# Expert rounds of a routed feed-forward kernel: counts, digits, turns and two vector operations at other places

## The chip, the cores and the metric

The kernel runs on one core of one Trainium2 chip. The metric is the device time of one execution in microseconds (us); lower is better. TensorE (PE) multiplies matrices, VectorE (DVE) and ScalarE (ACT) work elementwise, GpSimd (POOL) also issues the indirect transfers, and SyncE (SP) issues plain transfers. Every engine runs its own instructions in the order in which they are written; between engines only semaphores order the work.

## The reference

```python
def reference(**kwargs):
    attn_out = _attn_ref(**attn_kwargs)              # linear attention, 4 x 8 heads x 768 tokens x 48
    x = attn_out ... reshape(3072, 384)
    x = _moe_ref(x=x, **moe_kwargs)                  # x @ w_in, leaky relu with slope alpha, @ w_out
    return _moe2_ref(x=x, **moe2_kwargs)

def _moe2_ref(x, w_gate, w1, w2):                    # N 3072, D 384, E 8 experts, F 1024
    cap = N // E                                     # 384 tokens for each expert
    order = np.argsort(-(x @ w_gate).flatten())
    for idx in order:                                # greedy: best (token, expert) pair first
        tok, e = (int(idx) // E, int(idx) % E)
        if assigned[tok] >= 0 or counts[e] >= cap:
            continue
        assigned[tok] = e
        counts[e] += 1
    for e in range(E):
        mask = assigned == e
        out[mask] = np.maximum(x[mask] @ w1[e], 0.0) @ w2[e]
```

The first two parts (attention and the first feed-forward layer) are not touched. This case is about the last part: 3072 tokens are handed out to 8 experts of 384 tokens each, and each expert is a feed-forward layer 384 -> 1024 -> 384.

## The kernel before

**Eight experts, one search ahead.** The greedy loop is replaced by eight searches. Search p finds which expert fills up next and at what threshold; its 384 tokens are then known, and are expert p of the stream. TensorE works on expert p while search p + 1 runs in the gaps. One such stretch is called a round: `body(new)` on TensorE, with `new` from 0 to 7. Round `new` carries search q = new + 1; search 7 (in round 6) is short, since only one expert is left.

**The stream.** A round has 48 places (`at` = 0 to 47). At each place TensorE issues one step of the stream, three matmuls with a moving size of 384 (L1312, L1313, L1314: each product is made of a high and a low float part). Groups of three places alternate between a hidden piece (`expert_hidden(p, f)`, x times w1, `xeh`/`xel` in the rows) and a back piece (`expert_back(p, f)`, hidden times w2, `gh`/`gl` in the rows), with f from 0 to 7. The stream lags by 15 places, so places 0 to 14 still belong to the expert before: place 0 starts the back piece of f = 4, place 3 the hidden piece of f = 6, place 6 the back piece of f = 5, and so on; place 15 starts the new expert's first hidden piece. After a hidden piece ACT makes the high part with a relu (`relu_hi`, L737), then VectorE the low part (`relu_lo`, L1113); the back piece of that f waits for it (`g2l_ready`).

**The search.** A search has six steps m = 1 to 6. In each VectorE compares all keys with 40 thresholds (the `grid`, L1203 or L1205), TensorE counts with 12 small matmuls (`count`, L1505), VectorE turns the counts into hits (`rest` L1210, `hits` L1211), TensorE makes one matmul of them (`digit`, L1552), and VectorE reads the threshold found (L1214). Only then can the next grid be made. After step 6 VectorE closes the search (`close`, with `running` L1223), TensorE makes `offsets` (L1556), VectorE the slots and the one-hot tiles `is_b` (L1147), TensorE `inverse` in two halves (L1564), VectorE the indices (`indices`, L1154). GpSimd then gathers the rows `xg` of the new expert with three indirect transfers (L589), and TensorE turns them (`turn_rows(new, a)`, a = 0 to 2, L1574) in the next round; ACT copies a turned piece to its high part (`rows_hi`, L743) and VectorE makes the low part `xel` (`rows_lo`, L1120). All three turned pieces of a round share one PSUM bank, so turn a waits for `rows_lo` of a - 1.

**What sets the order.** On TensorE, tables of places in `body`: `counts_at` and `digits_at` (one place for each of six steps), `offsets_at`, `inverses_at`, `turns_at`. At one place the order is count, digit, offsets, inverse, turn, and then the stream's step. On VectorE the order is written out in `route(p)`, and the low parts are fitted in by `while_counting(p, m)` (between a step's grid and its wait for the count) and `while_placing(p, m)` (between its hits and its wait for the digit):

```python
                    while_counting(p, level * V3 + n + 1)
                    dve.wait_ge(counts_done, m)
                    ...                              # rest, hits
                    while_placing(p, level * V3 + n + 1)
                    dve.wait_ge(digit_ready, m)
```

For p of 3 and more, `rows_lo(p - 1, 0)` stands in `while_counting` of step 2, `rows_lo(p - 1, 1)` in `while_placing` of step 2, and `rows_lo(p - 1, 2)` in `while_counting` of step 3. In these names the first number of a turned piece or a low part counts experts, and a search p works beside expert p - 1.

Of the kernel before, what the change touches and what calls it, by code (L numbers as in the profile page):

```python
# [32 lines left out]
def build(nc, rT, kT, rN, kN, v, wT, uR, w_in, w_out, alpha, w_gate, w1, w2, out):  # L33
# [3 lines left out]
    E, _, F2 = w1.shape  # L37
    KD = DM // P
    NF, NF2 = F // P, F2 // P
    NT = NCH * B  # L40
# [9 lines left out]
    with ExitStack() as ctx:  # L50
# [3 lines left out]
        def sem(name):  # L54
            return ctx.enter_context(nc.semaphore(name))
# [139 lines left out]
        onehot_ready, grid_ready, counts_done = sem("onehot_ready"), sem("grid_ready"), sem("counts_done")  # L195
# [84 lines left out]
        def hidden_h(p, f):  # L280

            return last_gh[:] if (p, f) == (E - 1, NF2 - 1) else gh[:, f % 2, 0:CAP]

        def hidden_l(p, f):

            return last_gl[:] if (p, f) == (E - 1, NF2 - 1) else gl[:, f % 2, 0:CAP]
# [511 lines left out]
        def _(dve):  # L798
# [137 lines left out]
            def over_experts(a):  # L936
                return a.unsqueeze(2).to_broadcast([P, a.shape[1], E])

            def over_tokens(a, n, m=NT):
                return a.unsqueeze(1).to_broadcast([P, m, n])  # L940
# [3 lines left out]
            def step(ins):  # L944

                ins.then_inc(route_step, 1)
                route_steps[0] += 1

            def hold(ins):

                step(ins)
                dve.wait_ge(route_step, route_steps[0])

            def front_best(js):

                hold(V.tensor_reduce(best[:, js], logits[:, js], AX_X, ALU.max))
                hold(V.tensor_tensor(onehot0[:, js], logits[:, js], over_experts(best[:, js]), ALU.is_equal))

            def front_rank(js):

                hold(V.tensor_tensor(ranked[:, js], onehot0[:, js], over_tokens(rev_ps, E, js.stop - js.start), ALU.mult))
                hold(V.tensor_reduce(rankmax[:, js], ranked[:, js], AX_X, ALU.max))
# [5 lines left out]
            def front_keys(js, done):  # L968

                V.tensor_tensor(onehot[:, js], ranked[:, js], over_experts(rankmax[:, js]), ALU.is_equal).then_inc(done, 1)  # L970
                hold(V.tensor_scalar(bits_s[:, js], best[:, js].bitcast(I32), 31, SIGN, ALU.arith_shift_right, ALU.bitwise_or))
                hold(V.tensor_tensor(bits_u[:, js], bits_s[:, js], best[:, js].bitcast(I32), ALU.bitwise_xor))
                step(V.tensor_copy(key_low[:, js], bits_u[:, js].bitcast(U16).rearrange("p (j h) -> p h j", h=2)[:, 0]))
# [136 lines left out]
            def relu_lo(p, f):  # L1110

                dve.wait_ge(g2h_ready, NF2 * p + f + 1)
                V.scalar_tensor_tensor(out=hidden_l(p, f), in0=banks[3 + f % 2][:, 0:CAP], scalar=0.0, in1=hidden_h(p, f).bitcast(F32),  # L1113
                                       op0=ALU.max, op1=ALU.subtract).then_inc(g2l_ready, 1)

            def rows_lo(p, a):

                dve.wait_ge(xgh_ready, NA * p + a + 1)
                rows = slice(a * P, (a + 1) * P)
                V.tensor_tensor(xel[:, p % 2, :, rows], turned_rows(p, a), xeh[:, p % 2, :, rows].bitcast(F32), ALU.subtract).then_inc(xgl_ready, 1)  # L1120
# [35 lines left out]
            def while_counting(p, m):  # L1156

                if p == 1 and m == 2:
                    rows_lo(0, 0)
                    rows_lo(0, 1)  # L1160
                if p == 1 and m == 4:
                    relu_lo(0, 0)
                if p == 2 and m == 2:
                    relu_lo(0, 6)
                    rows_lo(1, 0)
                if p == 2 and m == 3:
                    rows_lo(1, 2)
                    relu_lo(0, 7)
                if p == 2 and m == 6:
                    relu_lo(1, 1)  # L1170
                if p >= 3 and m == 1:
                    relu_lo(p - 2, 5)
                if p >= 3 and m == 2:
                    rows_lo(p - 1, 0)
                if p >= 3 and m == 3:
                    relu_lo(p - 2, 6)
                    rows_lo(p - 1, 2)
                if p >= 3 and m == 4:
                    relu_lo(p - 2, 7)
                if p >= 3 and m >= 5:  # L1180
                    relu_lo(p - 1, m - 5)

            def while_placing(p, m):

                if p == 1 and m == 2:
                    rows_lo(0, 2)
                if p == 2 and m == 4:
                    relu_lo(1, 0)
                if p >= 2 and m == 2:
                    rows_lo(p - 1, 1)  # L1190
                if p == 1 and m >= 5:
                    relu_lo(0, m - 4)
# [37 lines left out]
            def slots(p):  # L1230

                dve.wait_ge(running_ready, p + 1)
                dve.wait_ge(offsets_done, p + 1)
                step(V.scalar_tensor_tensor(out=sure_slot[:], in0=running[:, 0:NT], scalar=banks[5][:, 0:1], in1=sure_tie[:, 0:NT], op0=ALU.add, op1=ALU.mult))
                hold(V.scalar_tensor_tensor(out=tie_slot, in0=running[:, NT:2 * NT], scalar=banks[5][:, 1:2], in1=sure_tie[:, NT:2 * NT], op0=ALU.add, op1=ALU.mult))
                hold(V.tensor_tensor(slot, sure_slot[:], tie_slot, ALU.add))
# [14 lines left out]
            def route(p):  # L1251

                search(p, 0, key[:])
                hold(V.scalar_tensor_tensor(out=key2[:], in0=key[:], scalar=found[0], in1=key_low, op0=ALU.subtract, op1=ALU.add))
                search(p, 1, key2[:])
                close(p)
                slots(p)
                inversion(p)
                if p in (1, 2):
                    relu_lo(p - 1, 3)  # L1260
                inversion_b(p)
                if p >= 3:
                    relu_lo(p - 1, 3)
                dve.wait_ge(inverse_ready, 3 * p + 2)
                front_best(slice(0, NT))
                indices(p)
                front_rank(slice(0, NT))
                if p >= 1:
                    relu_lo(p - 1, 4)
                if p + 2 < E:  # L1270
                    front_keys(slice(0, NT), onehot_ready)
                survivors()
                if p + 2 < E:
                    start_key(slice(0, NT))
                if p == 1:
                    relu_lo(0, 5)
# [30 lines left out]
        def _(pe):  # L1307
# [308 lines left out]
            def body(new):  # L1616

                q = new + 1
                counts_at = ((2, 5, 18, 23, 27, 31), (7, 11, 15, 19, 23, 27), (3, 7, 12, 17, 21, 25))[new] if new < 3 else (2, 7, 11, 16, 21, 25)
                digits_at = ((4, 6, 19, 24, 28, 32), (9, 13, 16, 20, 24, 28), (5, 10, 14, 18, 22, 26))[new] if new < 3 else (4, 9, 13, 17, 22, 26)  # L1620
                offsets_at = (36, 32)[new] if new < 2 else 30
                inverses_at = ((44, 45), (40, 41))[new] if new < 2 else (38, 39) if new < E - 2 else (25, 26)
                turns_at = ((4, 4, 5), (9, 11, 13), (7, 9, 11))[new] if new < 3 else (5, 7, 10)
                busy_at = {0: 9, 2: 2, 4: 4, 5: 2, 6: 1, 7: 1} if new == 0 else {}
                for at in range(6 * NF2):
                    if q < E - 1:
                        for m in range(2 * V3):
                            if at == counts_at[m]:
                                count(q, m + 1)
                            if at == digits_at[m]:  # L1630
                                digit(q, m + 1)
                        if at == offsets_at:
                            offsets(q)
                        if at in inverses_at:
                            inverse(q, inverses_at.index(at))
                    elif q == E - 1:
                        if at == 2:
                            offsets(q)
                        if at in inverses_at:
                            inverse(q, inverses_at.index(at))  # L1640
                    for a in range(NA):
                        if at == turns_at[a]:
                            turn_rows(new, a)
                    busy(busy_at.get(at, 0), banks[0])
                    while done[0] < 6 * NF2 * new + at + 1 - BEGINS:
                        stream(done[0])
                        done[0] += 1
# [52 lines left out]
```

## Time and profile before

| | us |
|---|---|
| median of 3 runs | 809.49 |
| lowest, highest run | 808.98, 809.88 |
| span of the profiled execution | 808.1 |
| TensorE matmul busy in it | 770.3 |
| VectorE busy | 500.5 |
| GpSimd busy | 474.9 |
| ScalarE busy | 220.1 |

The profiled execution has no device time of its own beside its span; the span is what its first and last instruction enclose, and it lies 1.39 us below the median of the three runs. The stretch of the change begins at about 575 us. Times of places in a round are given by the trace's clock; a start of one three-matmul step to the next takes about 0.52 us where nothing is waited for.

### The profile page before, as it was taken

To read this page: it belongs to the slowest core of one execution; us is meant where nothing else is said; L and a number is where in the kernel's file an instruction comes from. 1 tells how busy PE (TensorE), PEld (TensorE's weight loads), DVE (VectorE), ACT (ScalarE), POOL (GpSimd) and SP (SyncE) were. 2 spreads that over 40 slices of the span, in tenths; PEclk is the share of its full clock that TensorE was granted. 3 is DMA by queue.
4 is the path that set the end of the run, shared out by engine and by line. 5 is a ranking of instruction groups with operands and counts; after the bars stand their busy time and mean duration, and the time that the engine had idled before them with its cause. 6 is when DMAs were issued, how large, how long until landed. Compare 5 with 4: busy or idle time off the path is not lost.

```text
span 808.1 us, 15970 instructions
## 1 busy us (share of the span) xinstructions
PE 770.3 (95%) x6320; PEld 649.6 (80%) x6320; DVE 500.5 (62%) x1038; ACT 220.1 (27%) x452; POOL 474.9 (59%) x471
## 2 busy tenths in 40 slices
PE   6899999999999999999999999939999999999997
PEld 4578888888888888888888888726887988989996
DVE  8877766556655565556655334477787777776221
ACT  1233322111211121112111211204244344353451
POOL 6899985555555555555554333107477775775871
PEclk8999999999999999999999999958999999999999
DMA  7865522222221222222000000014523605517401
GB/s 213 228 197 155 150 70 70 69 69 70 67 67 63 66 67 63 64 64 67 11 11 11 11 11 10 14 54 168 186 74 144 215 20 198 171 45 272 159 11 49
DMA packets 46569, 75.17 MB, mean 93 GB/s; under 512 B 6256, under 2 KB 31856, under 8 KB 46496
## 3 DMA queue, kind: packets, MB, share of 16 engines
q1 hardware_dynamic: 37776, 56.07, 22.1%
q10 hardware_dynamic: 5584, 8.46, 3.7%
q0 software_dynamic: 3136, 9.64, 3.4%
q8 instruction: 50, 0.82, 0.5%
q14 instruction: 23, 0.19, 0.1%
HBM read 64.71 MB, written 9.44 MB: 92 GB/s over the span
## 4 chain that ended last, share of the span: by engine, by line
PE 81%; DVE 11%; POOL 2%; issue 2%; ACT 2%; DMA 1%; SPq 0%; POOLq 0%; DVEq 0%; ACTq 0%
PE bank L1312 23%; PE bank L1314 22%; PE bank L1313 21%; PE bank L1329 3%; PE bank L1363 3%; PE bank L1346 2%; DVE grid L1205 2%; PE bank L1422 2%; PE bank L1505 2%; DVE grid L1203 1%; POOL gl L493 1%; PE bank L1564 1%; DVE both L860 1%; PE bank L1382 1%; DVE xel L1120 1%
## 5 line engine op out<-in xcount | busy, mean ns | idle before, releaser
L493 POOL TENSOR_TENSOR gl<-g,gh 128x512 fp32r<-128x512 f32 x96 | 128.2, 1336 | 202.4 <-ACT gh L667 202.2
L1003 DVE TENSOR_SCALAR q<-bank,alpha_sb 128x512 f32<-128x512 f32 x96 | 71.9, 749 | 146.2 <-PE bank L1314 146.0
L667 ACT CAST gh<-g 128x512 fp32r<-128x512 f32 x96 | 59.6, 621 | 335.4 <-PE bank L1314 298.8
L1312 PE MATMUL bank<-gh,wout_h 128*128 128x512 f32 x288 | 118.7, 412 | 1.2 <-DVE vs L887 0.4
L1312 PE MATMUL bank<-xTh,win_h 128*128 128x512 f32 x288 | 113.1, 393 | 0.3 <-DVE xTl L896 0.3
L1314 PE MATMUL bank<-gh,wout_l 128*128 128x512 f32 x288 | 112.8, 392 | 0.0
L1313 PE MATMUL bank<-gl,wout_h 128*128 128x512 f32 x288 | 112.4, 390 | 0.0
L1314 PE MATMUL bank<-xTh,win_l 128*128 128x512 f32 x288 | 112.2, 389 | 0.0
L1313 PE MATMUL bank<-xTl,win_h 128*128 128x512 f32 x288 | 112.0, 389 | 0.0
L599 POOL TENSOR_TENSOR w1l<-raw,w1h 128x384 fp32r<-128x384 f32 x64 | 65.1, 1016 | 38.4 <-ACT w2h L731 37.9
L1312 PE MATMUL bank<-xeh,w1h 128*128 128x384 f32 x192 | 69.6, 362 | 0.0
L1006 DVE SCALAR_TENSOR_TENSOR g<-bank,q 128x512 f32<-128x512 f32 x96 | 66.4, 691 | 3.3
L1312 PE MATMUL bank<-w2h,gh 128*128 128x384 f32 x189 | 68.0, 360 | 0.1
L1312 PEld LDWEIGHTS bank<-gh,wout_h 128*128 128x128 f32 x288 | 54.1, 188 | 14.7 <-POOL gl L493 2.6
L600 POOL TENSOR_TENSOR w2l<-raw,w2h 128x384 fp32r<-128x384 f32 x64 | 64.9, 1015 | 0.0
L1314 PE MATMUL bank<-xeh,w1l 128*128 128x384 f32 x192 | 64.7, 337 | 0.0
L1313 PE MATMUL bank<-xel,w1h 128*128 128x384 f32 x192 | 64.4, 336 | 0.0
L1313 PE MATMUL bank<-w2l,gh 128*128 128x384 f32 x189 | 63.8, 338 | 0.0
L1314 PEld LDWEIGHTS bank<-gh,wout_l 128*128 128x128 f32 x288 | 54.0, 188 | 12.1
L1314 PE MATMUL bank<-w2h,gl 128*128 128x384 f32 x189 | 63.7, 337 | 0.0
L1312 PEld LDWEIGHTS bank<-xTh,win_h 128*128 128x128 f32 x288 | 54.1, 188 | 11.8 <-DVE xTl L896 0.8
L1314 PEld LDWEIGHTS bank<-xTh,win_l 128*128 128x128 f32 x288 | 54.1, 188 | 11.5
(203 smaller groups left out, 1453.6 us busy)
## 6 DMA issues: line engine op xcount, KB each, us to landing
raw<-w SPq DMA_DIRECT2D x32, 768.0 KB
rt<-rT SPq DMA_DIRECT2D x48, 96.0 KB, 2.9
vs<-v SPq DMA_DIRECT2D x48, 96.0 KB, 3.0
vn<-v SPq DMA_DIRECT2D x24, 192.0 KB, 2.9
x2rows<-x2n SPq DMA_DIRECT2D x23, 192.0 KB, 1.9
kt<-kT SPq DMA_DIRECT2D x44, 96.0 KB, 2.5
kn<-kN SPq DMA_DIRECT2D x20, 192.0 KB, 2.5
rn<-rN SPq DMA_DIRECT2D x20, 192.0 KB, 2.6
```

Source lines behind the costliest of these rows:

```text
L493: nc.gpsimd.tensor_tensor(gl[:, f % 2], g[:, f % 2], gh[:, f % 2].bitcast(F32), ALU.subtract).then_inc(gl_ready, 1)
L599: nc.gpsimd.tensor_tensor(w1l[:, f], raw1[:, p % 2, :, f * P:(f + 1) * P], w1h[:, f].bitcast(F32), ALU.subtract).then_inc(wlo1_ready, 1)
L600: nc.gpsimd.tensor_tensor(w2l[:, f], raw2[:, p % 2, f, :], w2h[:, f].bitcast(F32), ALU.subtract).then_inc(wlo_ready, 1)
L667: nc.scalar.copy(gh[:, f % 2], g[:, f % 2]).then_inc(gh_ready, 1)
L1003: nc.vector.tensor_scalar(q[:, f % 2], h, 0.0, alpha_sb[:, f:f + 1], ALU.min, ALU.mult).then_inc(q_ready, 1)
L1006: nc.vector.scalar_tensor_tensor(out=g[:, f % 2], in0=h, scalar=0.0, in1=q[:, f % 2], op0=ALU.max, op1=ALU.add).then_inc(g_ready, 1)
L1205: V.scalar_tensor_tensor(out=grid[:, js, 0:R], in0=wide, scalar=found[level], in1=row, op0=ALU.subtract, op1=ALU.is_ge).then_inc(grid_read ...
L1312: nc.tensor.matmul(o, a_h, b_h, start=first, stop=False)
L1313: nc.tensor.matmul(o, a_h, b_l, start=False, stop=False)
L1314: return nc.tensor.matmul(o, a_l, b_h, start=False, stop=last)
L1329: mm = nc.tensor.matmul(score_bank(c, b, j)[halves(j), h * HT:(h + 1) * HT], kt[heads_in(j), b % 2, h], weights(c, b)[heads_in(j), j, h], ...
L1363: return nc.tensor.matmul(y_bank(c, b)[halves(j), cols], weights(c, b)[:, j, h], vs[:, b, j, cols], start=(h == 0), stop=(h == H - 1), ski ...
```

## The change

Four edits, all in the expert rounds. (1) In `route(p)`, the next search's keys (`front_keys`, four VectorE operations, L970 to L973) stand ahead of the low part of the fifth hidden piece, `relu_lo(p - 1, 4)`. This holds for every p from 1 to 5. (2) For searches 3 to 6, `relu_lo(p - 2, 7)`, the low part of the expert's last hidden piece (called the seventh in the change's short title, f = 7 here), moves from the count of step 4 to between the hits and the digit of step 3. (3) In rounds 2 to 5, counts, digits, offsets and inverses stand up to two places later. (4) The turns of round 2 stand one place later, and the first turn of rounds 3 to 6 one place earlier.

```diff
@@ while_counting
                 if p >= 3 and m == 3:
                     relu_lo(p - 2, 6)
                     rows_lo(p - 1, 2)
-                if p >= 3 and m == 4:
-                    relu_lo(p - 2, 7)
                 if p >= 3 and m >= 5:
                     relu_lo(p - 1, m - 5)
@@ while_placing
                 if p == 2 and m == 4:
                     relu_lo(1, 0)
+                if p >= 3 and m == 3:
+                    relu_lo(p - 2, 7)
@@ route
                 front_rank(slice(0, NT))
+                if p + 2 < E:
+                    front_keys(slice(0, NT), onehot_ready)
                 if p >= 1:
                     relu_lo(p - 1, 4)
-                if p + 2 < E:
-                    front_keys(slice(0, NT), onehot_ready)
                 survivors()
@@ body
-                counts_at = ((2, 5, 18, 23, 27, 31), (7, 11, 15, 19, 23, 27), (3, 7, 12, 17, 21, 25))[new] if new < 3 else (2, 7, 11, 16, 21, 25)
-                digits_at = ((4, 6, 19, 24, 28, 32), (9, 13, 16, 20, 24, 28), (5, 10, 14, 18, 22, 26))[new] if new < 3 else (4, 9, 13, 17, 22, 26)
-                offsets_at = (36, 32)[new] if new < 2 else 30
-                inverses_at = ((44, 45), (40, 41))[new] if new < 2 else (38, 39) if new < E - 2 else (25, 26)
-                turns_at = ((4, 4, 5), (9, 11, 13), (7, 9, 11))[new] if new < 3 else (5, 7, 10)
+                counts_at = ((2, 5, 18, 23, 27, 31), (7, 11, 15, 19, 23, 27), (4, 8, 12, 17, 21, 26))[new] if new < 3 else (2, 7, 12, 17, 21, 26)
+                digits_at = ((4, 6, 19, 24, 28, 32), (9, 13, 16, 20, 24, 28), (6, 10, 14, 18, 23, 28))[new] if new < 3 else (4, 9, 14, 18, 23, 28)
+                offsets_at = (36, 32)[new] if new < 2 else 31
+                inverses_at = ((44, 45), (40, 41))[new] if new < 2 else (39, 40) if new < E - 2 else (25, 26)
+                turns_at = ((4, 4, 5), (9, 11, 13), (8, 10, 12))[new] if new < 3 else (4, 7, 10) if new < E - 1 else (5, 7, 10)
```

The number of instructions on every engine stays as it was. Three places show the new order.

VectorE at the end of a search (edit 1), as a piece of the difference; L961 and L962 rank the experts for the next search, L1113 is the low part, L970 to L973 are the keys, and L1240 begins `survivors`:

```order
 L961 TENSOR_TENSOR ranked<-onehot,bank 128x192
 L962 TENSOR_REDUCE bank<-ranked 128x24
-L1113 SCALAR_TENSOR_TENSOR gl<-bank,gh 128x384
 L970 TENSOR_TENSOR onehot<-ranked,bank 128x192
 L971 TENSOR_SCALAR bits_s<-bank 128x24
 L972 TENSOR_TENSOR bits_u<-bits_s,bank 128x24
 L973 CAST bank<-bits_u 128x24
+L1113 SCALAR_TENSOR_TENSOR gl<-bank,gh 128x384
 L1240 TENSOR_SCALAR middle<-bank 128x24
 L1241 SCALAR_TENSOR_TENSOR middle<-bank,middle 128x24
```

The low part moved behind the four operations of the keys.

VectorE around steps 3 and 4 of searches 3 to 6 (edit 2), again as a piece of the difference; the first L1210 and L1211 are `rest` and `hits` of step 3, L1214 reads the threshold after the digit, L1203 is the grid of step 4:

```order
 L1210 TENSOR_TENSOR rest<-cap_c,bank 40x8
 L1211 TENSOR_TENSOR hits<-bank,rest 40x8
+L1113 SCALAR_TENSOR_TENSOR gl<-bank,gh 128x384
 L1214 TENSOR_REDUCE bank<-bank 128x1
 L1254 SCALAR_TENSOR_TENSOR key<-key,bank 128x24
 L1203 TENSOR_TENSOR grid<-key,bank 128x24x40
 L1207 SCALAR_TENSOR_TENSOR rev<-bank,rev 128x8
-L1113 SCALAR_TENSOR_TENSOR gl<-bank,gh 128x384
 L1210 TENSOR_TENSOR rest<-cap_c,bank 40x8
 L1211 TENSOR_TENSOR hits<-bank,rest 40x8
```

The low part now stands between the hits and the read of the threshold of step 3.

TensorE in round 2, search 3. Before, from the second turn (L1574) to the digit of step 2 (L1552) and the third turn; the three-row groups between are steps of the stream, and the count of step 3 comes one stream step after the last row:

```order
L1574 MATMUL bank<-id_wg,xg 128x128 x3
L1312 MATMUL bank<-xeh,w1h 128x384
L1313 MATMUL bank<-xel,w1h 128x384
L1314 MATMUL bank<-xeh,w1l 128x384
L1552 MATMUL bank<-hits,sized 128x8
L1312 MATMUL bank<-xeh,w1h 128x384
L1313 MATMUL bank<-xel,w1h 128x384
L1314 MATMUL bank<-xeh,w1l 128x384
L1574 MATMUL bank<-id_wg,xg 128x128 x3
```

The same stretch of the changed kernel, from the digit of step 2 to the count of step 3 (L1505) and the third turn:

```order
L1552 MATMUL bank<-hits,sized 128x8
L1574 MATMUL bank<-id_wg,xg 128x128 x3
L1312 MATMUL bank<-xeh,w1h 128x384
L1313 MATMUL bank<-xel,w1h 128x384
L1314 MATMUL bank<-xeh,w1l 128x384
L1312 MATMUL bank<-xeh,w1h 128x384
L1313 MATMUL bank<-xel,w1h 128x384
L1314 MATMUL bank<-xeh,w1l 128x384
L1505 MATMUL bank<-onehot,grid 128x16 x12
L1574 MATMUL bank<-id_wg,xg 128x128 x3
```

The second turn went from one stream step ahead of the digit to right behind it, and the third turn from one stream step ahead of the count to right behind it.

## Rows read from the trace of the kernel before

**Rows 1.** The page: span, and busy time of TensorE.

```profile
span 808.1 us, 15970 instructions
PE 770.3 (95%) x6320; PEld 649.6 (80%) x6320; DVE 500.5 (62%) x1038; ACT 220.1 (27%) x452; POOL 474.9 (59%) x471
```

**Rows 2.** Waits from 555 to 808 us: total us, times, longest us.

```profile
PEld bank L1505 <- DVE grid L1205: 4.5, 16, 0.7
```

**Rows 3.** Timeline at the end of round 0: start us, us, engine, line, operation, idle before.

```profile
575.89 0.56 DVE L1113 SCALAR_TENSOR_TENSOR gl<-bank,gh 128x384 fp32r<-128x384 f32 x1
576.37 0.34 DVE L970 TENSOR_TENSOR onehot<-ranked,bank 128x192 bf16<-128x192 f32 x1
577.15 0.17 DVE L1240 TENSOR_SCALAR middle<-bank 128x24 f32<-128x24 f32 x1
576.50 0.44 PE L1312 MATMUL bank<-w2h,gh 128*128 128x384 f32 x1
```

**Rows 4.** Timeline at the end of round 1.

```profile
606.91 0.34 DVE L1154 TENSOR_SCALAR idx<-bank 64x3 int32<-64x3 f32 x2 [1.57 <-PE bank L1564]
608.07 0.56 DVE L1113 SCALAR_TENSOR_TENSOR gl<-bank,gh 128x384 fp32r<-128x384 f32 x1
609.21 0.34 PE L1312 MATMUL bank<-w2h,gh 128*128 128x384 f32 x1
611.49 0.45 PE L1505 MATMUL bank<-onehot,grid 128*128 128x16 bf16 x12 [0.52 <-DVE grid L1203]
```

**Rows 5.** Timeline of round 2, steps 2 to 4 of search 3.

```profile
614.63 0.46 PE L1505 MATMUL bank<-onehot,grid 128*128 128x16 bf16 x12 [0.35 <-DVE grid L1205]
616.81 0.16 DVE L1211 TENSOR_TENSOR hits<-bank,rest 40x8 bf16<-40x8 f32 x1
616.73 0.52 PE L1574 MATMUL bank<-id_wg,xg 128*128 128x128 f32 x3 [0.21 <-DVE xel L1120]
617.79 0.56 DVE L1120 TENSOR_TENSOR xel<-bank,xeh 128x384 fp32r<-128x384 f32 x1 [0.82 <-ACT xeh L743]
618.47 1.22 DVE L1205 SCALAR_TENSOR_TENSOR grid<-key,bank 128x960 bf16<-128x960 f32 x1
619.74 0.46 PE L1505 MATMUL bank<-onehot,grid 128*128 128x16 bf16 x12 [0.20 <-DVE grid L1205]
623.29 0.46 PE L1505 MATMUL bank<-onehot,grid 128*128 128x16 bf16 x12
```

**Rows 6.** TensorE timeline of round 3, search 4; the last row opens round 4.

```profile
644.04 0.46 PE L1505 MATMUL bank<-onehot,grid 128*128 128x16 bf16 x12
650.63 0.34 PE L1314 MATMUL bank<-xeh,w1l 128*128 128x384 f32 x1
651.01 0.46 PE L1505 MATMUL bank<-onehot,grid 128*128 128x16 bf16 x12
654.41 0.46 PE L1505 MATMUL bank<-onehot,grid 128*128 128x16 bf16 x12
661.03 0.34 PE L1314 MATMUL bank<-w2h,gl 128*128 128x384 f32 x1
661.48 0.18 PE L1552 MATMUL bank<-hits,sized 65*128 65x8 bf16 x1
663.69 0.18 PE L1556 MATMUL bank<-running,before_b 128*128 128x2 bf16 x1
675.65 0.46 PE L1505 MATMUL bank<-onehot,grid 128*128 128x16 bf16 x12
```

**Rows 7.** TensorE timeline of round 6, at its second turn.

```profile
741.77 0.34 PE L1314 MATMUL bank<-w2h,gl 128*128 128x384 f32 x1
742.38 0.52 PE L1574 MATMUL bank<-id_wg,xg 128*128 128x128 f32 x3 [0.27 <-DVE xel L1120]
```

**Rows 8.** Gathered rows: the first gather of expert 4, and landing times of those recorded.

```profile
670.56 0.98 POOL L589 DMA_INDIRECT xg<-x2rows,idx  x1 [3.56 <-DVE idx L1154]
DMA to landing us min/median/max: 3.8/5.5/6.1
```

## The prediction, made before the changed kernel ran

> **What bounds the kernel now.** I read the page first: TensorE's matmuls are busy for 770.3 of 808.1 us [rows 1], so a change in the rounds counts only by what TensorE waits. Next the list of waits from 555 us on. It shows only short ones, the largest group being counts that wait for a grid, 4.5 us in 16 waits [rows 2]. Then the timelines, where I looked at start-to-start distances on TensorE: three matmuls of a stream step start 0.17 to 0.18 us apart, so any larger distance is an inserted matmul or a wait. Rounds 3, 4 and 5 are copies of each other: from the first count at 644.04 to the next round's at 675.65 are 31.61 us [rows 6]. In them TensorE waits before the count of step 3 (0.38 us from the matmul at 650.63 to 651.01, against 0.17: 0.21), by the same reading 0.24 before the count of step 4 at 654.41, about 0.08 before its digit, and 0.28 before the last digit (661.03 to 661.48, 0.45 against 0.17) [rows 6]. That is 0.8 us a round, the most that edit 3 can win there. The count and everything behind it stand in one chain: grid, count, hits, digit, read, next grid. A table that puts them later wins where TensorE came too early, and costs nothing as long as the chain keeps its own pace.
>
> **Edit 1, rounds 0 and 1: keys first.** At the end of round 0, VectorE makes the low part at 575.89, it ends at 576.45, and TensorE's back piece starts at 576.50 [rows 3]: TensorE is waiting for just this operation. The four key operations take from 576.37 to 577.15, 0.78 us [rows 3]. Put ahead, they delay the low part and so TensorE by 0.78. What VectorE does for the first grid is as long as before, and nothing later in round 1 waits for a clock of its own (grids, hits and turns all follow TensorE's count), so I take the whole 0.78 as lasting. The bounds are 0, if a later wait took it up, and 0.78. **+0.78.**
>
> At the end of round 1 the low part starts at 608.07 and the back piece runs at 609.21 [rows 4]. With keys first, the low part starts at 608.85, ends at 609.41, and TensorE starts at 609.46, 0.25 late, and 0.1 more for the refill that a first matmul behind a stall shows (0.28 to the next instead of 0.18). The first count then stands one place later. Before it was held to 611.49 by its grid [rows 4]; now four stream steps from 609.46 (0.63 and three of 0.53, the last of them place 3) bring it to 611.67, when the grid is done. The count is 0.18 later, but with one stream step more behind it. The 1.57 us that VectorE waits ahead of 606.91 [rows 4] is longer than the 0.65 us from an inverse to its indices in other rounds would make it; I can't explain it, and it favours the later first count.
>
> **Edits 3 and 4, round 2.** (Times in the clock of before, without the 0.78.) After the first digit the chain sets the second count as before: digit 613.12, grid from 613.55, count at 614.82 instead of 614.63 [rows 5]. The first turn follows it, as before. Hits of step 2 start 0.19 later than at 616.81 [rows 5], at 617.00. Now the new order bites. Before, the second turn ran at 616.73, ahead of the digit, its low part at 617.79, and the grid at 618.47 [rows 5]. VectorE makes that low part between hits and the read of the digit, so the read needs the turn. Now the turn stands behind the digit, which can't start before hits are done, 0.22 behind their start: 617.22. The turn starts at 617.30, its low part 1.06 later (616.73 to 617.79) at 618.36, the read and grid 0.68 behind that (617.79 to 618.47), at 619.05, and the third count 1.27 behind the grid's start, at 620.32 instead of 619.74 [rows 5]. TensorE would have been there at 618.70, so it waits 1.6 us. The third turn before ran ahead of the count, out of everyone's way; now it runs behind the count, at 620.7. Its low part, 1.06 behind by the same distance, is at 621.75 and takes 0.56 [rows 5], and VectorE makes it ahead of `rest`, which takes 0.2 more. So hits start at 622.50, the digit at 622.72, 0.6 later than TensorE would be. Edit 2 adds the low part of f = 7 there: started with 0.08 behind the start of hits, it lets the read start at 623.04, 0.10 later than the digit would. Key, grid and latency take 1.70 more: the fourth count at 624.74, where before it stood at 623.29, at the same place [rows 5]: **+1.45**, boundary of round 1 included.
>
> **Second half, rounds 2 to 5.** With counts at 17, 21, 26 and digits at 18, 23, 28, the chain allows each at or just before TensorE's arrival: from digit to next count the chain needs 1.70, and three stream steps give 0.04 + 0.61 + 0.53 + 0.53 = 1.71. The last digit gives up its wait of 0.28. But `offsets` stands three steps behind it, and the running sum is ready 1.94 behind the digit; before, four steps covered this (661.48 to 663.69, 2.21 [rows 6]). Three give 1.70, so a new wait of 0.25 comes. From the fourth count at place 17 to place 31 that makes 9.24 us. In round 2, before needed 9.45 for the same, and one inserted start (0.085) more is accounted by then: +1.45 - 0.21 + 0.08 = **+1.32** for round 2.
>
> In rounds 3 to 5: count 3 one place later finds its grid done (wins 0.21), and the low part of edit 2, ready at 652.0, is done before the read, so it costs nothing there and clears the wait of the next digit (0.08). Digit 3 and count 4 both move, and the wait between them stays, 0.22. The last digit wins 0.28, offsets lose 0.25, and the first turn shares a place with a digit (0.02 to 0.05 won). Carried through place by place from 644.04, place 31 starts at 663.88 instead of 664.36 (0.67 behind the offsets of [rows 6]); 0.085 comes off, the slower first start behind an insert, which before has already paid: 0.40 a round, three rounds: **-1.20**. Edit 1 is free here: in these rounds VectorE waits for ACT ahead of the fifth low part anyway, and the keys fill that wait. But the first count, at place 2 as before, had no wait to give.
>
> **Round 6.** The second turn waits 0.43 us (741.77 to 742.38, 0.61 against 0.18) for the first piece's low part [rows 7]. With the first turn one place earlier this is gone: **-0.43**.
>
> **Sum:** 0.78 + 1.32 - 1.20 - 0.43 = +0.47. The profiled execution's span becomes 808.1 + 0.47 = 808.6. The span lies 1.39 below the median of 809.49, and I keep that distance: 809.96, so **810.0 us**. This is within 0.2% (1.6 us), about what a measurement of this kernel can tell from no change.
>
> **The gathered rows.** The first turn at place 4 asks for rows earlier: issue at 670.56 + 0.13, turn at 676.76, which allows 6.07 us in rounds 4 and 5, and 5.74 in round 6. Landings recorded, of the third gather of a round, took 3.8 to 6.1, median 5.5 [rows 8]. So zero to 0.4 us is at stake in a round; I take zero, as the median is below both. The Trainium skill (DMA: Bandwidth & Descriptors, "Anatomy of one DMA — SWDGE (gpsimd) path") gives about 2.0 us fixed plus the bytes at 436 GB/s; for 192 KB that is an estimate of 2.5 us, and would leave over 3 us of slack. The recorded landings are over twice that beside the weight loads, so the row decides, and the page alone would hide this risk.
>
> **Rivals.**
> - *The turns in round 2 don't bind* (another order of release, or gathers and copies quicker than read): then round 2 wins like the others, its waits before counts 1 and 3, turns and last digit, some 1.0 to 1.3 less what offsets and edit 1 cost: -0.8 instead of +1.32. Sum -1.65: 807.8 us, on the faster side. For it speaks only that before shows five waits there to win; against it the order in the code. It decides if the third count waits under 0.3. Chance 0.13.
> - *Gathered rows come late.* If the first gather takes 6.6 us, rounds 3 to 5 wait 0.5 each and round 6 0.9: +2.4, with the sum 812.4; at 6.1 only +0.4. It decides from a landing of 6.1 on. Taken as 811.6. Chance 0.12.
> - *The tight steps don't fit.* 1.70 against 1.71 leaves nothing. Counts 5 and 6 each waiting 0.15 in four rounds cost 1.2: 811.2. Chance 0.12.
> - *The 0.78 is taken up later* by a wait in round 1 or 2: 809.2. Chance 0.15.
> - The forecast as summed: 0.48.
>
> **How the numbers follow.** Leaving out the faster rival's end and the far end of the late rows gives 808.3 to 811.3. Faster by over 0.2%: 0.08 of the first rival and 0.02 of the rest, 0.10. Slower: 0.07 of late rows, 0.06 of tight steps, 0.02 of the forecast, 0.15. Same: 0.75.
>
> **What would show it.** Right: the back piece at the end of round 0 starts near 577.3; in round 2 the third count idles over 1 us for its grid, with the second turn behind the digit; rounds 3 to 5 take 31.2 us from first count to first count; offsets wait 0.2 for `running`; round 6 has no wait at its second turn. Wrong: a wait on the first turn that ends with a transfer; rounds 3 to 5 at 31.6; a third count of round 2 without a wait.

## The result, and the profile after

| | before | after |
|---|---|---|
| median, 20 runs each | 809.36 us | 810.75 us |
| span of the profiled execution | 808.1 us | 809.7 us |

The ratio after to before is 1.0020, with a 95% interval of 1.0014 to 1.0027: the change costs 1.1 to 2.2 us. The forecast was 810.0.

The page of the changed kernel, span and busy times, beside [rows 1]:

```profile
span 809.7 us, 15957 instructions
PE 766.4 (95%) x6312; PEld 649.2 (80%) x6320; DVE 500.2 (62%) x1038; ACT 220.4 (27%) x452; POOL 476.0 (59%) x471
```

Busy times say nothing here. The work is the same; this trace merely lacks records that the other has (13 in all, 8 of them matmuls). What helps is a clock that both kernels share: the start of a given stream step. I take the start of the step at place 42, where no edit inserts or removes anything between one round and the next, and subtract. This gives the length of each round in the two traces, with the forecast of its difference:

| round | before | after | difference | forecast |
|---|---|---|---|---|
| 1 | 34.32 | 35.15 | +0.83 | +0.78 |
| 2 | 33.78 | 35.07 | +1.29 | +1.32 |
| 3 | 31.61 | 31.25 | -0.36 | -0.40 |
| 4 | 31.59 | 31.26 | -0.33 | -0.40 |
| 5 | 31.61 | 32.07 | +0.46 | -0.40 |
| 6 | 28.11 | 27.90 | -0.21 | -0.43 |
| 7 | 26.56 | 26.56 | 0.00 | 0 |

The sum is +1.68 (forecast +0.47); the stretch ahead of round 1 differed by -0.13 between the two traces. Rounds 1 to 4 came as forecast. Rounds 5 and 6 together are 1.08 us worse than forecast.

**Round 1.** The timeline at the end of round 0 of the changed kernel, beside [rows 3]:

```profile
575.75 0.35 DVE L970 TENSOR_TENSOR onehot<-ranked,bank 128x192 bf16<-128x192 f32 x1
576.54 0.55 DVE L1113 SCALAR_TENSOR_TENSOR gl<-bank,gh 128x384 fp32r<-128x384 f32 x1
577.15 0.44 PE L1312 MATMUL bank<-w2h,gh 128*128 128x384 f32 x1 [0.90 <-DVE gl L1113]
```

The keys take the place that the low part had, the low part starts 0.79 us behind them, and TensorE starts right at its end, 0.65 later on the trace's clock, in a trace that was 0.13 ahead.

**Round 2.** TensorE and VectorE around steps 2 to 4 of search 3, beside [rows 5]:

```profile
615.41 0.46 PE L1505 MATMUL bank<-onehot,grid 128*128 128x16 bf16 x12 [0.32 <-DVE grid L1205]
617.80 0.18 PE L1552 MATMUL bank<-hits,sized 65*128 65x8 bf16 x1 [0.51 <-DVE hits L1211]
617.90 0.52 PE L1574 MATMUL bank<-id_wg,xg 128*128 128x128 f32 x3
618.97 0.56 DVE L1120 TENSOR_TENSOR xel<-bank,xeh 128x384 fp32r<-128x384 f32 x1 [1.23 <-ACT xeh L743]
619.65 1.22 DVE L1205 SCALAR_TENSOR_TENSOR grid<-key,bank 128x960 bf16<-128x960 f32 x1
620.92 0.46 PE L1505 MATMUL bank<-onehot,grid 128*128 128x16 bf16 x12 [1.46 <-DVE grid L1205]
622.32 0.56 DVE L1120 TENSOR_TENSOR xel<-bank,xeh 128x384 fp32r<-128x384 f32 x1 [0.98 <-ACT xeh L743]
623.32 0.18 PE L1552 MATMUL bank<-hits,sized 65*128 65x8 bf16 x1 [0.51 <-DVE hits L1211]
625.33 0.46 PE L1505 MATMUL bank<-onehot,grid 128*128 128x16 bf16 x12 [0.16 <-DVE grid L1203]
```

Read downwards, this is the forecast chain: the digit waits for hits, the turn runs 0.10 behind it, its low part 1.07 later, the grid behind that, and TensorE has been idle for 1.46 us when the third count starts. From the second count to the fourth are 9.92 us; before it was 8.66 [rows 5].

**Rounds 3 to 5.** The first counts of these rounds, and the offsets that open round 6, beside [rows 6]:

```profile
646.03 0.46 PE L1505 MATMUL bank<-onehot,grid 128*128 128x16 bf16 x12
677.28 0.46 PE L1505 MATMUL bank<-onehot,grid 128*128 128x16 bf16 x12
708.54 0.46 PE L1505 MATMUL bank<-onehot,grid 128*128 128x16 bf16 x12
740.61 0.18 PE L1556 MATMUL bank<-running,before_b 128*128 128x2 bf16 x1
```

31.25 and 31.26, and then 32.07. The difference stands in two rows: the chain that ended last names the gather, which for once is longer than the stretch that covered it, and the first turn of round 5 in the timeline waits for it:

```profile
703.97 6.80 DMA xg<-x2rows,idx
```

```profile
710.81 0.55 PE L1574 MATMUL bank<-id_wg,xg 128*128 128x128 f32 x3 [0.65 <-DMA xg<-x2rows,idx]
```

The forecast put the first turn 6.07 us behind the issue and took zero wait; this gather needed 6.80.

### The profile page after: what moved, and what is told of

Same layout as the page of the kernel before. It is cut to its first block, busy times and chain, and to the rows that moved or that the text cites. A ratio compares the mean times of both kernels' runs of the same rounds, so it can differ in the third digit from the quotient of the medians.

```text
span 809.7 us, 15957 instructions
## 1 busy us (share of the span) xinstructions
PE 766.4 (95%) x6312; PEld 649.2 (80%) x6320; DVE 500.2 (62%) x1038; ACT 220.4 (27%) x452; POOL 476.0 (59%) x471
## 4 chain that ended last, share of the span: by engine, by line
PE 81%; DVE 11%; POOL 2%; issue 2%; DMA 1%; ACT 1%; another core or an unknown queue 0%; POOLq 0%; SPq 0%; DVEq 0%; ACTq 0%
PE bank L1312 23%; PE bank L1314 21%; PE bank L1313 21%; PE bank L1363 3%; PE bank L1329 3%; PE bank L1346 2%; PE bank L1422 2%; PE bank L1505 2%; DVE grid L1205 1%; POOL gl L493 1%; DVE both L860 1%; PE bank L1574 1%; DVE grid L1203 1%; PE bank L1564 1%; DMA xg<-x2rows,idx 1%
```

## The experiments

The experiments ran in three sets, each on a chip of its own, so each time is given as a ratio to the runs of before in the same set. The medians of before were 808.0, 809.07 and 808.25 us there, and 809.36 beside the result above. The round lengths come from the profiles, as above.

One thing differs between the sets, and it bears on every comparison of round 2. At the end of round 1, VectorE needs the second `inverse` for its indices (L1154). From the start of the one to the start of the other it took 1.36 to 1.96 us in the profiles of the result, 1.35 to 1.39 in all four of the set with 809.07, and 0.65 in all eight of the other two sets, whatever the kernel. I call the first late and the second prompt indices. The first row is the changed kernel's, whose second inverse started at 605.64; the second comes from the run with the first turn of rounds 3 to 6 back at 5 (below), whose second inverse started at 605.70 and which is the same program up to the end of round 2:

```profile
607.02 0.34 DVE L1154 TENSOR_SCALAR idx<-bank 64x3 int32<-64x3 f32 x2 [0.98 <-PE bank L1564]
606.35 0.34 DVE L1154 TENSOR_SCALAR idx<-bank 64x3 int32<-64x3 f32 x2 [0.25 <-PE bank L1564]
```

Round 2 of the changed order took 35.07 us with late and 34.86 with prompt indices. No profile of the kernel before has prompt ones; the run with edit 1 alone has, and its round 2 took 33.12 against 33.78 and 33.85; edit 1 doesn't change round 2 (first experiment), so I take this as an estimate for the old tables. So round 2 is compared below between profiles of one kind.

**Keys first only from search 3 on.**

```diff
-                if p + 2 < E:
+                if p + 2 < E and p >= 3:
                     front_keys(slice(0, NT), onehot_ready)
                 if p >= 1:
                     relu_lo(p - 1, 4)
+                if p + 2 < E and p < 3:
+                    front_keys(slice(0, NT), onehot_ready)
```

> The changed kernel, with the old order of keys and fifth low part for searches 1 and 2 alone (keys first only from search 3 on). Theory (the back piece at the end of round 0 waits for just this low part): the 0.65 to 0.78 us of round 0 come back and nothing else moves, so about 810.0 us against 810.75 of the changed kernel, and round 1 starts its place 0 near 576.4 us. Rival (the delay is taken up by a later wait, or the median doesn't show it): 810.7 us.

Round 1 took 34.34 us instead of 35.15: the 0.8 us are this operation's. Its place 0 started at 575.69, in a trace that was 0.81 ahead of the first one of before, where it stood at 576.50. Nothing of them is taken up later: round 2 took 34.88, and 34.86 in the run of the same set that has keys first there (first turn back at 5, below), both with prompt indices. The time was 809.56 against 808.0, ratio 1.0015 (1.0006 to 1.0024). The changed kernel had 1.0020, with late indices, and the intervals overlap. The profile shows the theory, the times don't contradict it and don't prove it.

**Turns of round 2 back at 7, 9, 11.**

```diff
-turns_at = (..., (8, 10, 12))[new]
+turns_at = (..., (7, 9, 11))[new]
```

> The changed kernel, with the turns of round 2 back at 7, 9, 11; its counts and digits stay at the new places. Theory (the turn behind the digit and the turn behind the count make VectorE late): the waits before the third count (1.5 us) and its digit (0.5 us) go, round 2 ends 0.4 to 0.6 us ahead of before instead of 1.3 behind, so about 809.0 us. Rival (the later counts themselves cost the time): 810.5 us, with the third count still waiting over 1 us.

Ratio 0.9992 (0.9983 to 1.0001), and round 2 took 32.39 us with prompt indices: 2.47 less than the 34.86 of the changed order, and 0.73 less than the 33.12 of the old tables. I expected 1.7 to 1.9 and 0.4 to 0.6. The wait ahead of the third count fell from 1.46 to 0.20:

```profile
618.23 0.46 PE L1505 MATMUL bank<-onehot,grid 128*128 128x16 bf16 x12 [0.20 <-DVE grid L1205]
```

So the later counts with the turns left at 7, 9, 11 are a gain, and the later turns turned it into a loss. But this isn't the order of before with everything shifted. Before, the second count and the first turn shared place 7, and the count (at 614.63, [rows 5]) came first:

```profile
614.95 0.53 PE L1574 MATMUL bank<-id_wg,xg 128*128 128x128 f32 x3
```

Here the count stands at place 8, and the first turn has come ahead of it (613.26, the count at 614.31).

**Which turn: two steps between.** (8, 9, 12), and then (8, 9, 11) in the same place.

> The changed kernel with the second turn of round 2 at place 9 instead of 10, so ahead of the digit of step 2; the first stays at 8, the third at 12. Theory (the read of step 2 waits for the low part of this turn): the third count stands 0.4 us earlier and round 2 takes 34.7 instead of 35.07. Rival (this turn alone carries the loss): round 2 near 33.0.

> The same with the third turn at place 11 too, so ahead of the count of step 3; the first stays at 8. Theory (hits of step 3 wait for the low part of this turn): another 0.9 us off, round 2 near 33.8; the rest down to the 32.4 of turns at 7, 9, 11 belongs to the first turn, which stands behind the second count. Rival (the third turn costs nothing): round 2 as in the run before it.

| turns of round 2 | round 2, us, prompt indices | step |
|---|---|---|
| 8, 10, 12 | 34.86 | |
| 8, 9, 12 | 34.45 | -0.41 |
| 8, 9, 11 | 33.60 | -0.85 |
| 7, 9, 11 | 32.39 | -1.21 |

The first line is the run with the first turn of rounds 3 to 6 back at 5 (below). The second turn gives 0.41 and the third 0.85, as worked out (0.4 and 0.9), and no rival stands. The first turn gives the most, 1.21, and this size nobody had worked out: behind the second count it makes VectorE late with `rest` of that step, and delays the second turn, which waits for its low part (0.73 us in the run with 8, 9, 12). Yet it stood behind that count before, too, so these 1.21 us are no part of the loss against before. They are a gain that the later counts open and that the first turn at 8 forgoes. With the order of before kept (8, 9, 11), round 2 took 0.48 more than the 33.12 of the old tables; the second and third turn behind the digit and the count make it 1.74. The wait of the second turn:

```profile
616.52 0.52 PE L1574 MATMUL bank<-id_wg,xg 128*128 128x128 f32 x3 [0.73 <-DVE xel L1120]
```

**First turn of rounds 3 to 6 back at 5.**

```diff
-(4, 7, 10) if new < E - 1 else (5, 7, 10)
+(5, 7, 10)
```

> The changed kernel, with the first turn of rounds 3 to 6 back at place 5. Theory (the gathered rows come late for place 4): no wait on a transfer in rounds 3 to 6; round 5 gets 0.8 us back, round 6 loses 0.2, so 810.1 us. Rival (that wait was an accident of the profiled execution and the median has none): the wait of 0.43 us at the second turn of round 6 is back and nothing is won, 811.1 us.

Ratio 1.0022 (1.0013 to 1.0031), no better than the 1.0020 of the changed kernel, though that was taken in another set. Round 5 fell from 32.07 to 31.54, not to 31.25: even at place 5 the turn waited 0.3 us for the transfer. Rounds 3 and 4 took 31.33 and 31.36, 0.1 more than at place 4, and round 6 28.09 with its old wait back. So the wait on gathered rows is real, but moving the turn is no good cure; the shared place with the digit was worth 0.1. This profile, and those of five other runs with the late counts and the weights as before, recorded the first gather too: for round 5 it took 6.75 to 6.88 us, for round 6 5.9 to 6.2, and for rounds 3 and 4 5.8 to 6.0.

**The kernel before and the changed one, profiled again.**

> The kernel before, unchanged, for a second profile. Theory (the traced waits are those of every execution): rounds of 34.3, 33.8, 31.6, 31.6, 31.6, 28.1 and 26.6 us again, from round 1 on. Rival (the 1.57 us that VectorE waits for the inverse at the end of round 1 is an accident of the first profile): round 2 takes 33.1 to 33.3 us, as its first count has no wait then, and the change costs 0.5 to 0.7 us more than the first pair of traces shows.

> The changed kernel, unchanged, for a second profile beside it. Theory: rounds of 35.1, 35.1, 31.25, 31.25, 32.0, 27.9 and 26.6 us again, with the wait of 0.7 us for gathered rows in round 5. Rival (that wait is an accident): round 5 at 31.25.

Before gave 34.35, 33.85, 31.62, 31.56, 31.58, 28.08 and 26.55; after 35.14, 35.05, 31.27, 31.25, 32.03, 27.83 and 26.55. Round lengths repeat within 0.08 us, though the stretch ahead of round 1 moved by 1.27 us between the two profiles of before. The late rows in round 5 are no accident (the wait on the transfer was 0.61 us this time). The indices were late in both, as in the first pair, so the rival on round 2 was not tested by these two. The run with edit 1 alone (below) tested it: 33.12, within the rival's 33.1 to 33.3. What comes ahead of the rounds makes most of the scatter, and it is the reason why round lengths tell more than a span.

**Edit 2 undone.**

```diff
                 if p >= 3 and m == 3:
                     relu_lo(p - 2, 6)
                     rows_lo(p - 1, 2)
+                if p >= 3 and m == 4:
+                    relu_lo(p - 2, 7)
@@ while_placing
-                if p >= 3 and m == 3:
-                    relu_lo(p - 2, 7)
```

> The changed kernel with edit 2 alone undone: the low part of f = 7 back at the count of step 4. Theory (in round 2 it delays the read by 0.1, in rounds 3 to 5 it clears 0.08 before the digit of step 4): round 2 shorter by 0.1, rounds 3 to 5 longer by 0.05 to 0.1, the sum no more than 0.3 us either way. Rival (this edit carries a cost of its own): round 2 shorter by 0.5 or more.

Round 2 took 35.07 (late indices, as in the changed kernel's profiles), unchanged and not 0.1 shorter, and round 3 31.36, 0.11 more. Round 4 took 31.57, 0.31 more, of which 0.2 stand between the first digit and the second count (2.20 us against 1.98), where the first turn is, and 0.1 behind the fourth count. So edit 2 wins 0.1 us a round where the steps are tight, and the lateness of the rows varies.

**Rows ahead of the second half of the weights.**

```diff
-                    if p == 0 and c == 1:
+                    if p < E - 1 and c == 1:
                         for a in range(NA):
-                            sp.wait_ge(gathered[a], 16)
+                            sp.wait_ge(gathered[a], 16 * (p + 1))
```

> The changed kernel, with the second half of each expert's weight load (experts 1 to 6) held back until the gathered rows of that expert have landed. Theory (the gather is slow because it shares the transfer engines with the weight load): the first turn at place 4 waits no longer, round 5 takes 31.25 instead of 32.07 and round 6 27.7 instead of 27.9, landings fall below 5.4 us; 1.0 us below the changed kernel, so the ratio to before is near 1.0006. Rival (the gather is slow by itself): round 5 stays at 32.0, and the weights' later arrival may add a wait of ScalarE.

Ratio 1.0011 (1.0001 to 1.0020). Round 5 took 31.26 and round 6 27.67, both as expected. The landing times of the recorded gathers, first of the changed kernel, then of this one:

```profile
DMA to landing us min/median/max: 3.5/5.3/5.8
```

```profile
DMA to landing us min/median/max: 3.0/3.1/4.1
```

So the gather is slow because the second half of the same expert's weights moves beside it. This settles the step that failed. Whether the two meet in the transfer engines, which were busy all the time from 701 to 709 us in the changed kernel, or in the memory behind them, no run separates.

**Edit 1 alone on the kernel before.**

> The kernel before with edit 1 alone (keys first in every search). Theory: round 1 takes 35.1 instead of 34.3 us, all other rounds stay within 0.1 of before, the time is 0.6 to 0.8 us above before, ratio 1.0007 to 1.0010. Rival (in rounds 3 to 5 the earlier grid also helps, since the first count at place 2 was just reached): 0.1 us a round back, ratio 1.0005.

Ratio 1.0009 (1.0000 to 1.0018). Round 1 took 35.12, +0.80, and rounds 3 to 6 stayed at 31.61, 31.60, 31.61 and 28.11: keys first gains nothing there. But round 2 took 33.12 against 33.78 and 33.85, where the theory had no change. This is not the edit's doing: both profiles of before had late indices, and TensorE waited 0.52 us for the first count in one and 0.39 for the first digit in the other; this run has prompt ones and no such wait. Between two profiles with prompt indices, edit 1 left round 2 alone (34.88 and 34.86, above). So edit 1 costs 0.8 us, and they stay; the ratio agrees. The other 0.66 to 0.73 are an estimate of what late indices cost the old tables, where the changed order loses only 0.2. From it follows an estimate for the whole change with prompt indices: +1.74 instead of +1.29 in round 2, so 2.1 us in all.

**Repairs together.** First with offsets at 32 and the first turn at 5 in rounds 3 to 5; then with the first turn at 4 and the gathered rows ahead of the second half of the weights.

```diff
-                offsets_at = (36, 32)[new] if new < 2 else 31
+                offsets_at = (36, 32)[new] if new < 2 else 32
-turns_at = (..., (8, 10, 12))[new] if new < 3 else (4, 7, 10) ...
+turns_at = (..., (7, 9, 11))[new] if new < 3 else (5, 7, 10) if new < E - 2 else (4, 7, 10) ...
```

> The three repairs together (keys first from search 3 on; turns of round 2 at 7, 9, 11; first turn of rounds 3 to 5 at 5, of round 6 at 4), and offsets of rounds 2 to 5 at place 32 instead of 31. Theory: round 1 level with before, round 2 ahead by 0.5, rounds 3 to 5 by 0.55 each (0.35 plus the offsets' wait of 0.25), round 6 by 0.2: 2.3 to 2.5 us below before, 807.0 us. Rival (offsets one place later delay the slots and the inverse, or give their wait to the inverse): rounds 3 to 5 at 0.35, 807.6 us.

> All repairs together: keys first from search 3 on, turns of round 2 at 7, 9, 11, offsets of rounds 2 to 5 at place 32, first turn of rounds 3 to 6 at place 4, and the second half of the weight load behind the gathered rows. Theory: rounds of 34.3, 32.1, 31.05, 31.05, 31.05, 27.7 and 26.6 us, 3.7 us less than before in sum, ratio to before about 0.9955. Rival (the wait for gathered rows hid another one, for weights or low parts, as ScalarE gets its second half later): rounds 3 to 5 at 31.3 or more, ratio 0.997.

The first has a ratio of 0.9968 (0.9956 to 0.9980) and rounds of 34.37, 32.13, 31.07, 31.10, 31.40, 28.15 and 26.57; in rounds 5 and 6 it still waits for rows. In sum they are 2.8 us less than before, and the medians (805.52 and 808.0) differ by 2.48, for 2.3 to 2.5 expected. The second has 804.79 against 808.25 us, ratio 0.9957 (0.9943 to 0.9970), and rounds of 34.33, 32.12, 30.99, 31.00, 31.00, 27.67 and 26.57: in sum 3.9 us less than before, each within 0.07 of its expectation. Against round 2 of the old tables with prompt indices, as this run has them, the sum is an estimate of 3.2 us; the medians differ by 3.46. Offsets one place later gave 0.26 a round (31.25 to 30.99), the wait of 0.25 that the forecast had put there. It is faster than the kernel before by more than the interval; the changed kernel did not run beside it. Its first turn of round 5 no longer waits:

```profile
704.69 0.53 PE L1576 MATMUL bank<-id_wg,xg 128*128 128x128 f32 x3
```

## Why the prediction was right, and where it was wrong

The measured 810.75 lies inside the range and 0.8 above the forecast, and the difference of the medians is 1.39 us where 0.47 was forecast. So the direction and most terms were right, and the width of the range, not the sum, took up a term that was wrong. A wait on the first turn that ends with a transfer was on the list of signs against the forecast, and it came.

- **Edit 1, the 0.78 as lasting:** right in size (0.83; 0.80 with the edit alone, and 0.81 come back with it undone), and right that it lasts: with prompt indices, round 2 took 34.86 with keys first and 34.88 without.
- **Boundary of round 1:** the low part with keys first was to make TensorE 0.25 late. It didn't (609.91 in the changed trace, 0.70 behind before, as all of round 1): TensorE was already 0.7 late, and VectorE's indices only 0.11. In place of it came a wait at the first digit, as ACT's high part of f = 5 came only at 612.17. The two nearly cancel.
- **Edits 3 and 4, round 2:** the mechanism was right, and +1.29 for +1.32. The digit behind hits, the third count and the fourth each started within 0.1 of the forecast, with round 1's delay of 0.65 added, and the two turns that the working blames carry 0.41 and 0.85. That the size came out so well has luck in it. The working starts from a trace in which the indices of round 1 were late, 1.57 us of wait that it couldn't explain, and the changed kernel was profiled with late indices too. With prompt ones the same edits cost 1.74 in round 2, and the sum would have fallen short by 1.7 us instead of 1.2. And it doesn't see that a first turn ahead of the second count was worth 1.21 us, which the forecast of this change did not need.
- **Second half and rounds 3 to 5:** -0.36 and -0.33 for -0.40; the new wait at offsets is there (the running sum holds them), and the tight steps fit to within 0.05.
- **The gathered rows: the step that failed.** "I take zero, as the median is below both." It measured 0.8 us in round 5 and 0.2 in round 6, 1.08 of the 1.2 us by which the sum of the rounds fell short. Two faults: the recorded landings were those of a round's third gather, while the first one, issued 2.6 us earlier in the middle of the weight load, took 6.80; and a median says nothing of the rounds that are late. In rounds 3 and 4 zero was right, but by a hair: six profiles show 5.8 to 6.0 us there against 6.07 allowed, and in one more (edit 2 undone) round 4 lost 0.2. The rival named the mechanism and its threshold of 6.1, at a chance of 0.12. That the weights make the gather slow was not only argued: with their second half held back, the median landing of the third gathers fell from 5.3 to 3.1 and the wait was gone. The Trainium skill's sum for one such transfer (DMA: Bandwidth & Descriptors, "Anatomy of one DMA — SWDGE (gpsimd) path"), by which 192 KB are an estimate of 2.5 us, comes near the 3.0 to 3.2 us without company, and misses the 6.80 with it by more than half.
- **Round 6, -0.43:** the wait at the second turn is gone, but 0.2 of it moved to the first turn, which waited for rows; with rows first, round 6 is 0.44 shorter.

## What to carry to other kernels

When a table of places is moved, follow every operation that an in-order engine has between the two events, not only the two events: here a copy between hits and read made the place of a turn more important than the place of the counts. An operation moved ahead of another costs its whole length wherever the second one is what the busiest engine waits for, even if it is free in all the rounds that look typical; so read the first and last rounds on their own. And a transfer that is asked for earlier needs its own landing time under its own load, at the worst of the rounds; where it moves beside a bulk load that isn't urgent, holding back the second half of that load is worth more than moving the consumer (1.1 us in rounds 3 to 6 here, against 0.2). Last, before a difference between two profiles is put down to an edit, look whether the stretch ahead of it ran alike in both: here a delay that went with the set of runs looked like 0.66 us won by an edit.

## What the runs showed of the hardware

An indirect gather of 192 KB landed in 3.0 to 3.2 us with the second half of the weights held back (rounds 1 to 6 of the last run, all but one gather, which took 3.45), and in 4.5 to 6.9 us beside a whole weight load. At the end of round 1, VectorE and ACT both started late on work of TensorE in 6 of 14 profiles. From the start of the second inverse to the indices it took 0.65 us in eight, 1.35 to 1.39 in five and 1.96 in one, and ACT's next relu started 1.30 us behind that inverse in the same eight and 1.94 to 2.07 in the other six, as here in the kernel before (inverse at 604.95):

```profile
606.89 0.49 ACT L737 ACTIVATE gh<-bank 128x384 fp32r<-128x384 f32 x1 [4.64 <-PE bank L1314]
```

It goes with the set of runs and not with the kernel, as told above. At the ends of rounds 2 to 5 the indices took 0.65 us in all 14 profiles, with the same kind of weight load beside them, so the load alone doesn't explain it. What holds the two engines there stays open; no run here took it apart.
